# The first pair of heads: scores from raw float32 operands in place of rounded and split ones

## The chip, the cores and the metric

The kernel runs on one core of one Trainium2 chip. The metric is the device time of one execution in microseconds (us). The core has five engines that run their own instruction streams and meet only at semaphores: TensorE (PE in the profile; its weight loads are PEld), VectorE (DVE), ScalarE (ACT), GpSimd (POOL) and SyncE (SP), which here only issues DMA transfers. Each engine works strictly in the order of its own stream.

## What is computed

Windowed attention with a distance bias over 4 batches x 8 heads, sequence 576, head size 64, and then two feed-forward layers on the result.

```python
scores = scale * np.matmul(q, k.transpose(0, 1, 3, 2))
mask = (rel >= 0) & (rel < window)                      # window 128
scores = np.where(mask, scores + bias[None], -1000000000.0)
scores = scores - np.max(scores, axis=-1, keepdims=True)
attn = np.exp(scores)
attn = attn / (np.sum(attn, axis=-1, keepdims=True) + 1e-09)
x = np.matmul(attn, v)                                  # to (2304, 512)
h = x @ w_in;  g = h * (1.0 / (1.0 + np.exp(-1.702 * h)));  x = g @ w_out
h = x @ w_in2; g = where(h >= 1, h, where(h <= -1, 0, (h + 1) ** 2 / 4)); out = g @ w_out2
```

Inputs and output are float32, the weights 512 x 2048 and 2048 x 512 in each layer.

## The kernel before

**Stages.** Attention runs first, to about 146 us of the span; the two layers, built of three-term products of rounded and remainder parts, fill the rest. The change touches only the first pair of heads in attention.

**Attention.** The 32 heads are taken in 16 pairs. A pair has five steps (`ITEMS`): four of them hold two score blocks of 128 queries x 256 keys, the fifth (`d == 0`) both heads' tails of 64 queries. The order of the steps is `FIRST_ORDER = (2, 4, 3, 0, 1)` in the first pair and `STEP_ORDER = (2, 3, 0, 1, 4)` afterwards, so there are 80 steps, counted by `m`; steps 0 to 4 are the first pair's. For step m, TensorE makes the scores (line 994), VectorE adds the bias and finds the maximum (lines 1597, 1603), ScalarE takes exponentials (1225, 1230), TensorE transposes them two steps later (1007), ScalarE copies the result out of PSUM (1265), and TensorE multiplies with the values four or five steps after m (1022, 1028). Each engine's stream is written as a loop over m, and this loop is the order: what is placed at step m is queued behind everything of the steps before. Scores go round a ring of three PSUM banks.

**Operands.** A score product is made of rounded operands (fp32r). `qk_raw` holds four slots (`SPLIT_RING`) of raw queries and keys, head h in slot h % 4. In a slot, the upper 64 partitions hold both, the lower 64 the keys again, with zeros where the queries stand. VectorE rounds all of it into `qk_hi` (1579). The remainder of the keys goes to `k_lo`, by GpSimd (886), that of the queries to the lower half of `qk_hi`, by GpSimd too (890), for heads 2 and 3 by VectorE (1582). Two products, with `qk_hi` and with `k_lo`, then give a score block over 128 rows.

**The first pair.** Heads 0 and 1 are loaded in pieces (`load_piece`, lines 574 and 575: the upper half, then the keys for the lower half). The first piece has 384 keys (`FIRST_COLS`) and is rounded and split on VectorE (1554, 1556, 1563), ScalarE (1249, 1254) and GpSimd (872, 878); the rest follows (1569, 1571). Meanwhile TensorE runs products on zeros, `warm_up`: `WARM_UP = 22` ahead of step 0's scores and `KEEP_WARM = 16` behind them (line 967).

**Loads.** SyncE issues the transfers in a fixed order: pieces of heads 0 and 1, then heads 2 to 7 (`load_operands`, lines 584 and 586), each followed by the values (591, 592) of the head two before. Head 4 reuses slot 0, head 5 slot 1, so `load_operands` waits for the splits of heads 0 and 1. The identity for transposes and the tail part of the distance table are issued by ScalarE (1216, 1217). ScalarE makes the bias tables of pair 1 behind the exponentials of step 3 (`make_bias`, lines 1236 and 1243).

Of the kernel before, what the change touches and what calls it, by code (L numbers as in the profile page):

```python
# [58 lines left out]
WARM_UP = 22  # L59
KEEP_WARM = 16  # L60
# [26 lines left out]
CLEARED = 6  # L87
# [26 lines left out]
def build(nc, qkT, v_main, v_tail, w_pairs, bias_table, identity, out):  # L114
# [9 lines left out]
    def f32(ap):  # L124
        return ap.bitcast(F32)
# [50 lines left out]
    first_odd_rounded = sem("first_odd_rounded")  # L176
    first_rounded = sem("first_rounded")
    first_split = [sem(f"first_split{e}") for e in range(2)]
    first_keys_split = sem("first_keys_split")
    rest_rounded = sem("rest_rounded")  # L180
# [105 lines left out]
    def piece_keys(tile, e, first):  # L286
        if e == 0:
            return piece(tile, 0, first)[:, 0]
        keys_at = KEYS_AT[1] + FIRST_COLS
        return tile[:, 1, KEYS_AT[1]:keys_at] if first else tile[:, 1, keys_at:WIDTH]  # L290

    def piece_queries(tile, e, first, rows):
        return piece(tile, 0, first)[rows, 1] if e == 0 else all_queries(tile, 1, rows)

    def piece_lo(e, first):
        return k_lo[:, e, 0:FIRST_COLS] if first else k_lo[:, e, FIRST_COLS:SEQ]
# [267 lines left out]
    def _(sp):  # L564
        def load_piece(e, first):
# [5 lines left out]
            source_keys = qkT[e, :, SEQ * e:SEQ * (e + 1)]  # L571
            source_keys = source_keys[:, 0:FIRST_COLS] if first else source_keys[:, FIRST_COLS:SEQ]
# [173 lines left out]
        load_piece(1, True)  # L746
        load_piece(0, False)
# [121 lines left out]
    def _(pool):  # L869
        def split_first_keys():  # L870
            pool.wait_ge(first_odd_rounded, 1)
            nc.gpsimd.tensor_tensor(piece_lo(1, True), piece_keys(qk_raw, 1, True), f32(piece_keys(qk_hi, 1, True)),
                                    ALU.subtract).then_inc(first_keys_split, 1)
            pool.wait_ge(first_keys_split, 1)

        def split_rest_keys():
            pool.wait_ge(rest_rounded, 2)
            nc.gpsimd.tensor_tensor(piece_lo(1, False), piece_keys(qk_raw, 1, False), f32(piece_keys(qk_hi, 1, False)),
                                    ALU.subtract).then_inc(qk_split[1], 1)
            pool.wait_ge(qk_split[1], 1)  # L880

# [57 lines left out]
        split_first_keys()  # L939
        split_rest_keys()  # L940
# [22 lines left out]
    def _(pe):  # L963
# [5 lines left out]
        def scores(m):  # L969
            q, d = ORDER[m]  # L970
            if q == 0:
                if d == 2:
                    pe.wait_ge(first_split[0], 2)
                elif d == 4:
                    pe.wait_ge(first_split[1], 1)
                    pe.wait_ge(first_keys_split, 1)
                elif d == 3:
                    for head in (0, 1):
                        pe.wait_ge(qk_split[head], splits(head))
            elif d in (2, 3):  # L980
# [16 lines left out]

        def transpose_probs(m):
            q, d = ORDER[m]
            gi = group_of(m)  # L1000
# [210 lines left out]
    def _(act):  # L1211
# [21 lines left out]
        def make_bias(pair):  # L1233

            for h in (2 * pair, 2 * pair + 1):
                nc.scalar.activation(bias_sb[:, h], distance[:, 0:BAND], ACT.Copy, scale=SLOPES[h]).then_inc(bias_made, 1)
                if h == 0:
                    round_first(1)
                if pair == 0:
                    round_rest(h)  # L1240
            if pair == 0:
                act.wait_ge(tail_distance_in, 16)
# [3 lines left out]
        def round_first(e):  # L1246

            act.wait_ge(first_in[e], 32)
            nc.scalar.activation(piece(qk_hi, e, True), piece(qk_raw, e, True), ACT.Copy).then_inc(first_odd_rounded, 1)

        def round_rest(e):

            act.wait_ge(qk_in[e], 32)
            nc.scalar.activation(piece(qk_hi, e, False), piece(qk_raw, e, False), ACT.Copy).then_inc(rest_rounded, 1)
# [54 lines left out]
        for m in range(ALL_STEPS + TRANSPOSE_LAG):  # L1309
# [5 lines left out]
            if m in (3, 6, 11):  # L1315
                make_bias((3, 6, 11).index(m) + 1)
# [225 lines left out]
    def _(dve):  # L1542
# [4 lines left out]
        for e in range(2):  # L1547
# [465 lines left out]
```

## Time and profile before

| | |
|---|---|
| median of 3 runs | 856.34 us (856.2 to 856.57) |
| profiled execution | 856.35 us |
| its span, first to last instruction | 854.6 us |
| granted TensorE clock, mean | 1.000 |
| TensorE busy | 847.7 us, 99% |
| VectorE busy | 709.4 us, 83% |
| ScalarE busy | 537.0 us, 63% |
| GpSimd busy | 120.9 us, 14% |

The profile names an engine, the line of the kernel, the operation, and the tile written and read. Times of the trace count from the start of the span. A matmul's duration in it is the way of a product through the array, so that products that follow each other overlap: the distance from one start to the next is what a product costs. "Idle before" is the time in which the engine had nothing to run ahead of a row, and what ended it. TensorE is busy nearly all of the span, and the places at which it is not lie in the first 20 us.

### The profile page before, as it was taken

The page shows a single profiled execution, that of the slowest core. Times are in us where ns is not written, and L with a number is a line of the kernel's source. Part 1 is how long each engine was busy: PE and PEld are TensorE (multiplying, and loading weights), DVE is VectorE, ACT ScalarE, POOL GpSimd, SP SyncE. Part 2 cuts the span into 40 slices and gives each one's busy share as a digit, 9 for nine tenths or more (in the row PEclk, how much of TensorE's full clock was granted, in tenths as well). Part 3 has the DMA queues.
Part 4 walks back from the last instruction along what each step waited for, and adds up shares of the span by engine and source line. Part 5 has one row for each costly group of instructions (what it writes and reads, how often), then busy time and mean ns, then how long its engine had stood idle before and what let it go on. Part 6 is the DMA issues. An engine that isn't in the chain of part 4 may idle for free.

```text
span 854.6 us, 15515 instructions
## 1 busy us (share of the span) xinstructions
PE 847.7 (99%) x5746; PEld 844.2 (99%) x5746; DVE 709.4 (83%) x981; ACT 537.0 (63%) x789; POOL 120.9 (14%) x84
## 2 busy tenths in 40 slices
PE   8999999999999999999999999999999999999998
PEld 8999999999999999999999999999999999999998
DVE  7888988786988966778998887989989788889784
ACT  6778777767775546768644456767465567665441
POOL 5788898000000000000000000000000000000000
PEclk9999999999999999999999999999999999999999
DMA  8888761667776337686764772687647643788822
GB/s 204 220 211 219 199 170 67 267 256 270 258 246 232 129 144 271 253 306 244 259 243 177 279 242 104 219 284 259 230 143 278 226 156 122 287 302 299 302 74 75
DMA packets 63257, 186.45 MB, mean 218 GB/s; under 512 B 7504, under 2 KB 14352, under 8 KB 59344
## 3 DMA queue, kind: packets, MB, share of 16 engines
q1 hardware_dynamic: 62896, 185.30, 63.5%
q8 instruction: 47, 0.77, 0.4%
q14 instruction: 26, 0.21, 0.1%
q10 hardware_dynamic: 288, 0.16, 0.1%
HBM read 113.09 MB, written 72.35 MB: 217 GB/s over the span
## 4 chain that ended last, share of the span: by engine, by line
PE 95%; DVE 1%; SPq 1%; POOL 1%; issue 1%; DMA 0%; ACT 0%; DVEq 0%; POOLq 0%
PE ps L1060 83%; PE ps L1028 5%; PE ps L994 3%; PE ps L1007 3%; PE ps L1022 1%; PE ps L1037 1%; DVE qk_hi L1579 0%; DMA qk_raw<-qkT 0%; DVE probs L1603 0%; POOL qk_hi L890 0%; POOL k_lo L886 0%; SPq L575 0%; SPq L574 0%; DVE heads_out L1616 0%; PE ps L1042 0%
## 5 line engine op out<-in xcount | busy, mean ns | idle before, releaser
L1060 PE MATMUL ps<-arena,w_first 128*128 128x384 f32 x1764 | 331.3, 336 | 0.0
L1060 PEld LDWEIGHTS ps<-arena,w_first 128*128 128x128 f32 x1764 | 310.8, 188 | 0.9 <-DVE arena L1711 0.5
L1060 PE MATMUL ps<-arena,w_rest 128*128 128x384 f32 x1260 | 240.3, 336 | 0.0
L1060 PEld LDWEIGHTS ps<-arena,w_rest 128*128 128x128 f32 x1260 | 220.2, 188 | 0.5 <-issue 0.2
L1711 DVE TENSOR_TENSOR arena<-raw_first,arena 128x768 fp32r<-128x768 f32 (+1 forms) x114 | 148.8, 1318 | 77.2 <-ACT arena L1303 77.2
L1303 ACT ACTIVATE arena<-raw_first 128x768 fp32r<-128x768 f32 (+1 forms) x120 | 131.9, 1117 | 45.7 <-DVE raw_first L1672 39.7
L1060 PE MATMUL ps<-w_rest,arena 128*128 128x256 f32 x945 | 132.4, 281 | 0.0
L1060 PEld LDWEIGHTS ps<-w_rest,arena 128*128 128x128 f32 x945 | 121.1, 189 | 0.1
L1060 PE MATMUL ps<-w_first,arena 128*128 128x256 f32 x567 | 88.0, 282 | 0.0
L1711 DVE TENSOR_TENSOR arena<-raw_rest,arena 128x1536 fp32r<-128x1536 f32 (+1 forms) x48 | 71.3, 1486 | 8.6 <-ACT arena L1303 8.4
L1060 PEld LDWEIGHTS ps<-w_first,arena 128*128 128x128 f32 x567 | 76.0, 189 | 0.0
L1303 ACT ACTIVATE arena<-raw_rest 128x1536 fp32r<-128x1536 f32 (+1 forms) x48 | 60.9, 1268 | 23.0 <-PE ps L1060 21.0
L1345 ACT ACTIVATE d1s<-ps 128x384 f32<-128x384 f32 (+2 forms) x72 | 35.3, 490 | 40.9 <-PE ps L1060 40.8
L1230 ACT ACTIVATE probs<-probs,neg_max 128x256 f32<-128x256 f32 (+1 forms) x128 | 54.0, 472 | 7.4 <-DVE neg_max L1603 7.4
L1603 DVE CUSTOM_DVE_ANT_0 probs<-ps,bias_sb 128x256 f32<-128x256 f32 (+1 forms) x128 | 44.7, 387 | 16.0 <-PE ps L994 11.3
L1028 PE MATMUL ps<-v_sb,probs_t 128*128 128x65 f32 x448 | 57.0, 268 | 0.5 <-DVE heads_out L1616 0.5
L1028 PEld LDWEIGHTS ps<-v_sb,probs_t 128*128 128x128 f32 x448 | 55.3, 191 | 0.9 <-issue 0.9
L1336 ACT ACTIVATE ps<-ps 128x384 f32<-128x384 f32 (+2 forms) x72 | 34.2, 477 | 30.1 <-PE ps L1060 28.9
L1635 DVE TENSOR_TENSOR wst<-wst 128x256 f32<-128x256 f32 (+1 forms) x90 | 48.5, 538 | 2.8
L1265 ACT ACTIVATE probs_t<-ps 128x512 f32<-128x512 f32 x64 | 37.8, 590 | 18.8 <-PE ps L1007 18.8
L994 PE MATMUL ps<-qk_hi 128*128 128x256 f32 x160 | 48.6, 325 | 0.5 <-DVE qk_hi L1571 0.3
L886 POOL TENSOR_TENSOR k_lo<-qk_raw,qk_hi 128x576 fp32r<-128x576 f32 x30 | 44.7, 1490 | 16.9 <-DVE qk_hi L1579 15.6
(118 smaller groups left out, 973.1 us busy)
## 6 DMA issues: line engine op xcount, KB each, us to landing
gd<-g SPq DMA_DIRECT2D x24, 1536.0 KB, 6.1
raw_rest<-gd SPq DMA_DIRECT2D x32, 768.0 KB, 5.3
wst<-w_pairs SPq DMA_DIRECT2D x32, 512.0 KB, 5.8
raw_first<-gd SPq DMA_DIRECT2D x16, 768.0 KB, 5.9
yd<-ust SPq DMA_DIRECT2D x6, 1536.0 KB, 6.3
qk_raw<-qkT SPq DMA_DIRECT2D x30, 288.0 KB, 4.0
wd<-ust SPq DMA_DIRECT2D x4, 1536.0 KB, 9.4
raw_first<-yd SPq DMA_DIRECT2D x4, 1536.0 KB, 6.5
```

What stands on the lines that cost most here:

```text
L886: nc.gpsimd.tensor_tensor(k_lo[:, slot], keys(qk_raw, head), f32(keys(qk_hi, head)), ALU.subtract).then_inc(qk_split[slot], 1)
L994: last = nc.tensor.matmul(place, queries, k[:, key0:key0 + BAND], start=n_pass == 0 and (d > 0 or i == 0), stop=n_pass == 1 and (d > 0 or ...
L1028: last = nc.tensor.matmul(o_slot(2 * blk + e), probs_t[:, gi % 2, col:col + P], v_sb[:, h + e, max(blk - 1, 0) + piece], start=piece == 0, ...
L1060: last = nc.tensor.matmul(to, stationary, moving, start=start and n == 0, stop=n == len(steps) - 1, skip_group_check=True)
L1230: last = nc.scalar.activation(at, at, ACT.Exp, bias=neg_max[:, col:col + 1], scale=-1.0)
L1265: nc.scalar.activation(probs_t[:, gi % 2], pt_bank[gi % 2], ACT.Copy).then_inc(pt_copied[gi % 2], 1)
L1303: nc.scalar.activation(operand(k, i)[:, 0], source(k, i), ACT.Copy).then_inc(hi_made, 1)
L1336: nc.scalar.activation(b_bank(D, pos), a_bank(D, pos), ACT.Copy).then_inc(seeded_b, 1)
L1345: nc.scalar.activation(d1(D, pos), d_bank(D, pos), ACT.Copy).then_inc(d_copied, 1)
L1603: last = nc.vector.tensor_tensor_reduce(out=to[:, 0:width], in0=bank[:, i * BAND:i * BAND + width], in1=bias_sb[:, h + e, BAND - width:BAN ...
L1635: nc.vector.tensor_tensor(to, a, b, ALU.subtract).then_inc(w_added, 1)
L1711: nc.vector.tensor_tensor(at[:, 1], source(k, i), f32(at[:, 0]), ALU.subtract).then_inc(lo_made, 1)
```

## The change

The scores of the first pair's five steps are made straight from `qk_raw`, in float32, from the 64 upper partitions: one product a block instead of two. All rounding and splitting of heads 0 and 1 goes (on VectorE, ScalarE and GpSimd), and with it the four transfers of their lower halves. Products on zeros stand in front (14 instead of 22) and behind each of the five steps (3, 3, 4, 3, 3, instead of 16 behind step 0). SyncE issues the identity. Head 4's and head 5's loads now wait for the scores of the last step that reads heads 0 and 1. The order of some steps changes: the bias tables of pair 1 are made at step 2 instead of 3, the tail bias of pair 0 at step 1, and VectorE casts heads 2 and 3 at steps 2 and 3, with the query split of head 3 one step behind its cast.

```diff
-WARM_UP = 22
-KEEP_WARM = 16
+WARM_UP = 14
+KEEP_WARM = (3, 3, 4, 3, 3)
...
-CLEARED = 6
+CLEARED = 8
...
     def piece(tile, e, first):
-        ap = tile[:, e]
+        ap = tile[UPPER, e]
...
     def splits(head):
         use = head // SPLIT_RING
-        return 2 * use + 2 - (1 if head % SPLIT_RING == 1 else 0) if head >= 0 else 0
+        return 2 * use + 2 - (2 if head % SPLIT_RING < 2 else 0) if head >= 0 else 0
+
+    def landings(head):
+        return 32 * (head // SPLIT_RING + 1) - (16 if head % SPLIT_RING < 2 else 0)
...
-            sp.dma_start(piece(qk_raw, e, first)[UPPER], source_piece).then_inc(landed, 16)
-            sp.dma_start(piece_keys(qk_raw, e, first)[LOWER], source_keys).then_inc(landed, 16)
+            sp.dma_start(piece(qk_raw, e, first), source_piece).then_inc(landed, 16)
 
         def load_operands(head):
             slot = head % SPLIT_RING
             if head - SPLIT_RING in (0, 1):
-                sp.wait_ge(first_split[slot], 2 - slot)
-            if head - SPLIT_RING == 1:
-                sp.wait_ge(first_keys_split, 1)
+                sp.wait_ge(scores_ready, last_use(head - SPLIT_RING) + 1)
...
         load_piece(1, True)
+        sp.dma_start(ident[:], identity).then_inc(ident_in, 16)
         load_piece(0, False)
...
-        split_first_keys()
-        split_rest_keys()
         for head in range(2, 2 * PAIR_COUNT):
             split_head(head)
...
+        def first_scores(m):
+            d = ORDER[m][1]
+            if d == 2:
+                pe.wait_ge(cleared, CLEARED)
+                pe.wait_ge(first_in[0], 16)
+            elif d == 4:
+                pe.wait_ge(first_in[1], 16)
+            elif d == 3:
+                for head in (0, 1):
+                    pe.wait_ge(qk_in[head], landings(head))
+            wait_past(pe, scores_biased, m + 1 - SCORE_RING)
+            bank = score_bank[m % SCORE_RING]
+            for i, (e, blk) in enumerate(ITEMS[d] or ((0, 4), (1, 4))):
+                key0 = KEYS_AT[e] + (max(blk - 1, 0) * P if blk < 4 else SEQ - BAND)
+                query0 = QUERIES_AT[e] + blk * P if blk < 4 else TAIL_AT[e]
+                place = bank[:, i * BAND:(i + 1) * BAND] if d else bank[:, 0:BAND]
+                last = nc.tensor.matmul(place, qk_raw[UPPER, e, query0:query0 + P], qk_raw[UPPER, e, key0:key0 + BAND],
+                                        start=d > 0 or i == 0, stop=d > 0 or i == 1)
+            last.then_inc(scores_ready, 1)
...
         for m in range(ALL_STEPS + DRAIN):
-            if m < ALL_STEPS:
+            if m < STEPS:
+                first_scores(m)
+                warm_up(KEEP_WARM[m])
+            elif m < ALL_STEPS:
                 scores(m)
-            if m == 0:
-                warm_up(KEEP_WARM)
-                pe.wait_ge(ident_in, 16)
...
-        act.wait_ge(first_in[0], 32)
+        act.wait_ge(first_in[0], 16)
         act.dma_start(distance[:, BAND:], bias_table[:, BAND:]).then_inc(tail_distance_in, 16)
-        act.dma_start(ident[:], identity).then_inc(ident_in, 16)
...
-            if m in (3, 6, 11):
-                make_bias((3, 6, 11).index(m) + 1)
+            if m == 1:
+                act.wait_ge(tail_distance_in, 16)
+                make_tail_bias(0)
+            if m in (2, 6, 11):
+                make_bias((2, 6, 11).index(m) + 1)
+                make_tail_bias((2, 6, 11).index(m) + 1)
...
         for e in range(2):
+            nc.vector.memset(qk_raw[UPPER, e, ZEROS_AT[e]:ZEROS_AT[e] + TAIL], 0.0).then_inc(cleared, 1)
...
-        round_first()
         for m in range(ALL_STEPS + COPY_TAIL_LAG - 1):
...
-            if m == 0:
-                split_first_queries(1)
-                split_rest()
-            if m in (1, 2):
-                round_head(m + 1)
+            if m in (2, 3):
+                round_head(m)
+            if m in (2, 4):
+                split_queries(m // 2 + 1)
```

The order of TensorE's stream at its start, before the change. `arena` is the tile of zeros, `ps` is PSUM.

```order
L967 MATMUL ps<-arena 128x256 x21
L994 MATMUL ps<-qk_hi 128x256 [waits first_split0]
L994 MATMUL ps<-k_lo,qk_hi 128x256
L994 MATMUL ps<-qk_hi 128x256
L994 MATMUL ps<-k_lo,qk_hi 128x256
L967 MATMUL ps<-arena 128x256 x16
L994 MATMUL ps<-qk_hi 128x256 [waits first_keys_split,first_split1,ident_in]
```

And after the change, from the same place on to the first transposes.

```order
L938 MATMUL ps<-arena 128x256 x13
L977 MATMUL ps<-qk_raw 128x256 [waits first_in0,cleared]
L977 MATMUL ps<-qk_raw 128x256
L938 MATMUL ps<-arena 128x256 x3
L977 MATMUL ps<-qk_raw 128x256 [waits first_in1]
L977 MATMUL ps<-qk_raw 128x256
L938 MATMUL ps<-arena 128x256 x3
L977 MATMUL ps<-qk_raw 128x256 [waits qk_in1,qk_in0]
L977 MATMUL ps<-qk_raw 128x256
L938 MATMUL ps<-arena 128x256 x4
L992 MATMUL ps<-ident,probs 128x128 [waits probs_ready,ident_in]
```

A step has two products instead of four, they wait for transfers instead of splits, and the products on zeros stand behind every step.

The order of SyncE's stream from head 3's load (slot 3) to head 5's (slot 1), before the change.

```order
L584 DMA qk_raw<-qkT 64x1152
L586 DMA qk_raw<-qkT 64x576
L591 DMA v_sb<-v_main 128x260
L592 DMA v_sb<-v_tail 64x65
L584 DMA qk_raw<-qkT 64x1152 [waits qk_split0,first_split0]
L586 DMA qk_raw<-qkT 64x576
L591 DMA v_sb<-v_main 128x260
L592 DMA v_sb<-v_tail 64x65
L584 DMA qk_raw<-qkT 64x1152 [waits qk_split1,first_keys_split,first_split1]
```

And the same places after the change.

```order
L568 DMA qk_raw<-qkT 64x1152
L570 DMA qk_raw<-qkT 64x576
L575 DMA v_sb<-v_main 128x260
L576 DMA v_sb<-v_tail 64x65
L568 DMA qk_raw<-qkT 64x1152 [waits scores_ready]
L570 DMA qk_raw<-qkT 64x576
L575 DMA v_sb<-v_main 128x260
L576 DMA v_sb<-v_tail 64x65
L568 DMA qk_raw<-qkT 64x1152 [waits scores_ready]
```

The order stays, but heads 4 and 5 now wait for the fifth count of `scores_ready`, the scores of step 4; ahead of this piece stand 10 transfers instead of 13.

## Rows read from the trace of the kernel before

**Rows 1.** The page's busy times: us, share of the span, instructions.
```profile
PE 847.7 (99%) x5746; PEld 844.2 (99%) x5746; DVE 709.4 (83%) x981; ACT 537.0 (63%) x789; POOL 120.9 (14%) x84
```

**Rows 2.** TensorE's waits, whole run: line, releaser, us in total, times, longest.
```profile
PE ps L967 <- DVE arena L1544: 1.4, 1, 1.4
PE ps L1007 <- ACT probs L1230: 1.4, 2, 1.2
```

**Rows 3.** TensorE by time: start us, us, engine, line, operation, tiles, idle before.
```profile
1.36 5.06 PE L967 MATMUL ps<-arena 128*128 128x256 f32 x22 [1.36 <-DVE arena L1544]
6.22 0.47 PE L994 MATMUL ps<-qk_hi 128*128 128x256 f32 x1
...
7.13 2.18 PE L967 MATMUL ps<-arena 128*128 128x256 f32 x16
...
14.45 0.66 PE L1007 MATMUL ps<-ident,probs 128*128 128x128 f32 x4 [1.17 <-ACT probs L1230]
14.87 0.36 PE L994 MATMUL ps<-qk_hi 128*128 128x256 f32 x1
...
24.69 0.38 PE L994 MATMUL ps<-qk_hi 128*128 128x256 f32 x1
...
32.76 0.36 PE L994 MATMUL ps<-qk_hi 128*128 128x256 f32 x1
```

**Rows 4.** The chain that ended last, by time: start us, us, what.
```profile
9.49 4.01 DMA qk_raw<-qkT
13.52 1.03 DVE qk_hi L1579
```

**Rows 5.** VectorE by time, the casts of heads 4 and 5.
```profile
17.43 0.76 DVE L1579 CAST qk_hi<-qk_raw 128x1152 fp32r<-128x1152 f32 x1
...
18.95 1.43 DVE L1579 CAST qk_hi<-qk_raw 128x1152 fp32r<-128x1152 f32 x1
```

**Rows 6.** GpSimd by time, the splits of heads 4, 5 and 7.
```profile
18.33 1.43 POOL L886 TENSOR_TENSOR k_lo<-qk_raw,qk_hi 128x576 fp32r<-128x576 f32 x1 [1.73 <-DVE qk_hi L1579]
19.84 1.81 POOL L890 TENSOR_TENSOR qk_hi<-qk_raw,qk_hi 64x576 fp32r<-64x576 f32 x1
21.73 1.42 POOL L886 TENSOR_TENSOR k_lo<-qk_raw,qk_hi 128x576 fp32r<-128x576 f32 x1
23.23 1.41 POOL L890 TENSOR_TENSOR qk_hi<-qk_raw,qk_hi 64x576 fp32r<-64x576 f32 x1
...
30.27 1.42 POOL L890 TENSOR_TENSOR qk_hi<-qk_raw,qk_hi 64x576 fp32r<-64x576 f32 x1
```

**Rows 7.** Products with values, by line: ns min/median/max, first and last start, forms.
```profile
L1028 PE MATMUL ps<-v_sb,probs_t x448: 218/275/295, 15.4 to 144.2; 128*128 128x65 f32 x150
L1022 PE MATMUL ps<-v_sb,probs_t x64: 272/273/278, 20.7 to 142.7; 128*128 128x130 f32 x64
```

**Rows 8.** ScalarE by time, the first bias and the roundings of raw pieces.
```profile
5.56 0.42 ACT L1236 ACTIVATE bias_sb<-distance 128x256 f32<-128x256 f32 x1 [3.32 <-DMA distance<-bias_table]
6.57 1.01 ACT L1249 ACTIVATE qk_hi<-qk_raw 128x960 fp32r<-128x960 f32 x1 [0.60 <-DMA qk_raw<-qkT]
...
8.54 0.36 ACT L1254 ACTIVATE qk_hi<-qk_raw 128x192 fp32r<-128x192 f32 x1
```

**Rows 9.** Transfers: all to 40 us; SyncE by time; landing, lines 574, 575; lower halves.
```profile
DMA packets 5908, 8.67 MB, mean 217 GB/s; under 512 B 1699, under 2 KB 4195, under 8 KB 5904
...
0.75 0.67 SPq L574 DMA_DIRECT2D qk_raw<-qkT  x1
...
11.34 0.52 SPq L584 DMA_DIRECT2D qk_raw<-qkT  x1
...
DMA to landing us min/median/max: 2.7/3.2/3.2
...
DMA to landing us min/median/max: 2.7/3.0/3.3
...
qk_raw<-qkT SPq DMA_DIRECT2D x11, 144.0 KB, 4.6
```

More of the change, by code:

```diff
@@ L175, in build @@
     first_in = [sem(f"first_in{e}") for e in range(2)]
[L176 to L180, printed above, removed]
     v_in = [sem(f"v_in{i}") for i in range(HEADS)]
@@ L284, in piece @@
         return ap[:, TAIL:keys_at] if first else ap[:, keys_at:WIDTH]
[L286 to L296, printed above, removed]
     def splits(head):
         use = head // SPLIT_RING
-        return 2 * use + 2 - (1 if head % SPLIT_RING == 1 else 0) if head >= 0 else 0
+        return 2 * use + 2 - (2 if head % SPLIT_RING < 2 else 0) if head >= 0 else 0
+    def landings(head):
+        return 32 * (head // SPLIT_RING + 1) - (16 if head % SPLIT_RING < 2 else 0)
     def last_use(head):
@@ L970, in scores @@
             q, d = ORDER[m]
[L971 to L980, printed above, removed]
+            if d in (2, 3):
                 head = 2 * q if d == 2 else 2 * q + 1
@@ L996, in scores @@
             last.then_inc(scores_ready, 1)
+        def first_scores(m):
[17 more added lines that the diff above has]
+            last.then_inc(scores_ready, 1)
         def transpose_probs(m):
             q, d = ORDER[m]
+            if m == 0:
+                pe.wait_ge(ident_in, 16)
             gi = group_of(m)
@@ L1236, in make_bias, with make_tail_bias @@
                 nc.scalar.activation(bias_sb[:, h], distance[:, 0:BAND], ACT.Copy, scale=SLOPES[h]).then_inc(bias_made, 1)
[L1237 to L1242, printed above, removed]
+        def make_tail_bias(pair):
             nc.scalar.activation(bias_tail[:, pair], distance[:, BAND:BAND + TAIL_KEYS], ACT.Copy,
                                  scale=SLOPES[2 * pair]).then_inc(bias_made, 1)
[L1246 to L1254, printed above, removed]
         def copy_pair(q):
@@ L1547, in _ @@
         for e in range(2):
+            nc.vector.memset(qk_raw[UPPER, e, ZEROS_AT[e]:ZEROS_AT[e] + TAIL], 0.0).then_inc(cleared, 1)
             nc.vector.memset(f32(qk_hi[:, e::2, ZEROS_AT[e]:ZEROS_AT[e] + TAIL]), 0.0).then_inc(cleared, 1)
         nc.vector.memset(half[:], 0.5).then_inc(cleared, 1)
-        def round_first():
-            dve.wait_ge(first_in[0], 32)
-            nc.vector.tensor_copy(piece(qk_hi, 0, True), piece(qk_raw, 0, True)).then_inc(first_rounded, 1)
-            dve.wait_ge(first_rounded, 1)
-            nc.vector.tensor_tensor(piece_lo(0, True), piece_keys(qk_raw, 0, True), f32(piece_keys(qk_hi, 0, True)),
-                                    ALU.subtract).then_inc(first_split[0], 1)
-            split_first_queries(0)
-        def split_first_queries(e):
-            if e:
-                dve.wait_ge(first_odd_rounded, 1)
-            nc.vector.tensor_tensor(piece_queries(qk_hi, e, True, LOWER), piece_queries(qk_raw, e, True, UPPER),
-                                    f32(piece_queries(qk_hi, e, True, UPPER)), ALU.subtract).then_inc(first_split[e], 1)
-        def split_rest():
-            dve.wait_ge(rest_rounded, 1)
-            nc.vector.tensor_tensor(piece_lo(0, False), piece_keys(qk_raw, 0, False), f32(piece_keys(qk_hi, 0, False)),
-                                    ALU.subtract).then_inc(qk_split[0], 1)
-            nc.vector.tensor_tensor(piece_queries(qk_hi, 0, False, LOWER), piece_queries(qk_raw, 0, False, UPPER),
-                                    f32(piece_queries(qk_hi, 0, False, UPPER)), ALU.subtract).then_inc(qk_split[0], 1)
         def round_head(head):
             slot, use = head % SPLIT_RING, head // SPLIT_RING
-            dve.wait_ge(qk_in[slot], 32 * (use + 1))
+            dve.wait_ge(qk_in[slot], landings(head))
             if use:
@@ L1579, in round_head, with split_queries @@
             nc.vector.tensor_copy(loaded(qk_hi, head), loaded(qk_raw, head)).then_inc(qk_rounded, 1)
-            if head in DVE_QUERIES:
-                dve.wait_ge(qk_rounded, head - 1)
-                nc.vector.tensor_tensor(all_queries(qk_hi, head, LOWER), all_queries(qk_raw, head, UPPER),
-                                        f32(all_queries(qk_hi, head, UPPER)), ALU.subtract).then_inc(qk_split[slot], 1)
+        def split_queries(head):
+            dve.wait_ge(qk_rounded, head - 1)
+            nc.vector.tensor_tensor(all_queries(qk_hi, head, LOWER), all_queries(qk_raw, head, UPPER),
+                                    f32(all_queries(qk_hi, head, UPPER)), ALU.subtract).then_inc(qk_split[head % SPLIT_RING], 1)
         def bias_scores(m):
```

12 lines of the change are left out of this document (removed).

## The prediction

> **What bounds the kernel now.** I read the page's busy shares first: TensorE is busy 847.7 of 854.6 us [rows 1]. Then its waits over the whole run: of four entries the two longest are 1.4 us in front of the first product on zeros and 1.4 us in front of transposes that want probabilities [rows 2], both before 19 us; the other two hold 0.8 us together. So a change at the start is worth what it brings forward the point from which TensorE never waits again, and no more. The list by time shows that point [rows 3]. 22 products on zeros run from 1.36 us, the first scores start at 6.22, 16 more products on zeros fill 7.13 to 9.31, and the last long wait (1.17 us, for the exponentials of step 2) ends at 14.45. Step 5's scores, the first of pair 1, start at 14.87, those of step 11 at 24.69. Neither kind of filler is work; it covers loads, casts and splits.
>
> What ends that start late? Head 3's second transfer, issued at 9.49 as the fifteenth of SyncE's queue, takes 4.01 us and releases the cast at 13.52 [rows 4, 5]. Behind it stand head 4 and 5's casts (17.43, 18.95) and GpSimd's splits: head 4's k_lo at 18.33, its queries at 19.84, head 5's at 21.73 and 23.23, ending 24.64 [rows 5, 6]. Step 11's scores, which need head 5, start 0.05 us later. So there are two chains with next to no slack at 24.69: TensorE's own work, and GpSimd's. The second is simple arithmetic: from the end of head 4's cast (17.43 + 0.76 = 18.19) to the end of head 5's splits (24.64) are 6.45 us.
>
> **Price of a raw product.** There is no such product of 256 columns in the trace. Its kin are the products of probabilities with values, which are float32 too: 448 records for the 224 products of the code (14 per pair, 16 pairs), so two records a product. With 65 columns the shortest record is 218 ns, with 130 columns the median is 273 [rows 7]: 55 ns for 65 columns, 0.85 ns a column, two columns' time at the higher level of 2.4 GHz. At 256 columns a record then holds the array for 256 x 0.85 = 0.22 us and a step of two products, four records, for 0.88 us, against 4 x 0.118 = 0.47 us for the rounded pair it replaces (its records start 0.12 us apart once fast). Bounds: 0.47 us (columns cost nothing more) and 1.75 us (twice the records). I take 0.88; both kinds of evidence point at it. Five steps: 5 x 0.41 = 2.1 us more TensorE work. At the lower level, 1.2 GHz, where a product on zeros takes 4.86/22 = 0.221 us, it is 0.43 us a record.
>
> **The clock.** The granted clock of the rows reads 1.00 throughout, but pace tells which level holds: 0.221 us a product until about 7.1, then some 0.12 [rows 3]. TensorE had by then been busy without a gap since 1.36. I keep 7.3 us as the change, since the new kernel is as gapless.
>
> **TensorE's own chain after.** Removed are 8 of 22 products on zeros, and the wait for cast and two subtractions; 14 x 0.221 from 1.36 ends at 4.45. The first transfer of head 0 alone is needed: issued at 0.75, at most 3.2 us to land, 3.95, so it is there. Scores 0: 4 x 0.43, to 6.17. Three on zeros: 6.83. Scores 1 (second piece, issued near 2.1, landed by 5.3): one slow record, three fast, 7.92. Zeros 8.27, scores 2 9.15 (pieces issued by 3.9, landed by 7.1), four on zeros 9.62, transposes 10.02 (step 0's probabilities: VectorE from 6.5 to 7.3, ScalarE to 8.1; the identity, issued near 2.6, has landed). Scores 3 10.90, zeros 11.25, transposes 11.65, scores 4 12.53 with its result at 12.7; zeros and transposes to 13.3. Step 5's scores thus start at 13.3 instead of 14.87: 1.57 us won. For this the exponentials of steps 1 and 2 must be done by 11.25 and 12.9; they end near 9.8 and 11.6, behind VectorE's 0.7 us and ScalarE's 0.9 us a step. ScalarE also loses its three roundings of raw pieces (1.01 us the longest, 0.36 the shortest, 1.9 together [rows 8]); pair 1's biases move from behind step 3's exponentials to behind step 2's, about 1 us of work where it now has room. The distance table, issued 0.63 us earlier, lets the first bias start near 4.9 instead of 5.56 [rows 8].
>
> Heads 2 and 3: SyncE issues four lower-half transfers fewer and one (identity) more, three issues of about 0.63 us, 1.9 us earlier at head 3. It is also bytes: the transfers up to head 3 hold about 2.1 MB before and 0.29 MB less after, and the queue moves about 0.22 MB per us [rows 9], so head 3 lands near 11.7 to 12.1, is cast by 12.8 and its k_lo ready at 14.8; step 6's scores come at 15.7. That covers it; if it fails, each us is lost there.
>
> **The new wait.** SyncE now holds head 4's load for the scores of step 4, the last readers of the raw slots 0 and 1. Queued behind it are head 4's second half, head 2's values, head 5 and everything up to head 7. Before, head 4 was issued at 11.34 [rows 9]. After: 12.75, second half 13.4. Bounds of the landing: at the start, with an empty queue, second halves took 2.7 to 3.3 us; over the first 40 us, with a full queue, 4.6 at the median [rows 9]. Nothing was issued for 3.3 us before it, so I take the former, plus 0.2 for 144 instead of 96 KB: landed at 16.6 (bounds 16.1 and 18.0). Cast 0.76: done at 17.35, against 18.19, that is 0.84 us earlier (bounds 1.3 earlier, 0.6 later). Plus 6.45 gives 23.8 for step 11, where TensorE alone would come at 24.69 - 1.57 = 23.1. GpSimd decides: TensorE waits about 0.7 us and has won 24.69 - 23.8 = 0.9 us. The values and heads queued behind come 1.4 us later, but their need is far off (head 6 issued at about 17.5 for a cast near 24).
>
> What of head 5? Issued at 15.15 and 15.8, it lands at 18.9 (800 KB to 1 MB behind one another at 0.22 MB per us) or up to 20.4. The cast of head 5 took 1.43 us beside GpSimd's split instead of 0.76 [rows 5], and head 4's queries beside it 1.81 instead of 1.41 [rows 6]. If it lands inside head 4's query split, the two together end some 0.3 us later: 24.1. I take 0.1 of that: a gain of 0.8 us, on the profile's own 856.35 us (span 854.6 and 1.75 around it), equal to the median of 856.34. **Forecast 855.5 us.** After step 11 all is TensorE again: head 7's splits end at 30.27 + 1.42 = 31.69 and step 16's scores, which need them, start at 32.76 [rows 3, 6], 1 us of slack that the 0.8 us doesn't use up, so the gain goes through to the end unchanged.
>
> The Trainium skill ("SBUF — State Buffer", section "SBUF: two separate sides") says that VectorE and GpSimd share a port pair under an exclusive lock, so that whichever starts second waits for the whole of the other. The trace agrees with a cast that lasts until the split beside it has ended. By that rule head 5's cast would wait from 18.9 to the end of head 4's queries at 20.4.
>
> **Rivals.**
> (a) *Full lock on head 5's cast.* It waits until 20.4, ends at 21.2, and GpSimd's two further operations end at 24.1: gain 0.6, less 0.1 for step 7's bias that stands behind it: 855.8. For: the 1.43 us row [rows 5]; the rule of "SBUF — State Buffer" in the Trainium skill, told above, would make it so. Against: before, the cast came first and the split gave way.
> (b) *Earlier clock.* If the level rises at 4.8, 2.5 us of slow pace become 1.25, step 4 ends at 11.4, and head 4 follows: gain 0.8 + 1.25, 854.3. The same comes out if raw products cost less. For: nothing fixes the moment to 7.3. Against: one profile and three times within 0.4 us.
> (c) *Head 4's load takes the 4.6 us of the full queue.* Landed 18.0, cast 18.76, 0.57 us later than before: 856.9. For: most rows. Against: the queue is empty then.
> (d) *Slower: the clock stays at the lower level.* Raw products use 64 of 128 rows, and now stand among few products on zeros. If the pace of 0.221 lasts beyond 7.3, every us costs 0.5; gone at 9.0 is the whole gain, and with step 4 all slow, 5.4 us are added at 12.7, less 0.8: 860.9. For: 20 records of a kind the trace has not. Against: no gap opens for it.
> (e) *Raw products need more records than two*, or fewer, against what the 448 records say: a step of 1.75 us would add 5 x 0.87 = 4.4 us before the end of step 4 and lead to about 860, one of 0.47 us lead to (b)'s time.
>
> **Chances.** Forecast 0.35 (own range 855.0 to 855.8), (a) 0.15, (b) 0.20, (c) 0.16, (d) 0.09, (e) 0.05. A measurement of this kernel can tell about 0.2%, 1.7 us. Faster than 854.6: most of (b) and half of (e), 0.19. Slower than 858.1: (d), half of (e) less a little, 0.12. Within: 0.69. The range leaves out (d) and the ends of (b) and (c): 854.1 to 857.5.
>
> **What would show it.** Right: the first raw product at 4.4 to 4.5, records 0.43 us apart and after 7.3 us 0.22 apart; step 4's scores ending near 12.7, head 4's transfer issued at once, its cast ending near 17.4; a wait of about 0.7 us of TensorE on GpSimd's split before step 11, at 23.8. Wrong: that wait missing or longer; a cast of head 3 that comes after 12.8; SyncE not idle between 9.4 and 12.7; pace 0.22 for products on zeros after 8 us; or two records of a raw product not 0.22 us apart.

## The result, and the profile after

The changed kernel is slower: 858.9 us at the median of 10 runs, against 856.4 of the kernel before (ratio 1.0051, 95% interval 1.0035 to 1.0066). That is half a per cent, and clear of the noise. Its times are not one cluster. Over the 16 times measured of it in this study, 8 lie at 864.09 to 864.71, 6 at 858.55 to 859.01, and 2 at 857.1 and 857.7; the kernel before lies at 855.97 to 857.00. Three executions of this study (1004 and 1391 us of the kernel before, 2148 us of own128nf below) lie far outside and stand in no comparison. A median between such clusters says little, so two traces are shown: the profiled run, at 864.51 us (span 862.7), and one more of the same kernel, look2, at 858.82 (span 857.0).

First the waits of TensorE in the run at 864.51: line, releaser, us in total, times, longest.

```profile
PE ps L938 <- DVE arena L1518: 1.4, 1, 1.4
PE ps L1013 <- DVE heads_out L1570: 0.8, 3, 0.3
```

It waits less than before: the 1.17 us for probabilities [rows 2, 3] are gone, as forecast. The time went elsewhere. TensorE by time in the same run (start us, us, engine, line, operation, tiles, count):

```profile
1.36 3.36 PE L938 MATMUL ps<-arena 128*128 128x256 f32 x14 [1.36 <-DVE arena L1518]
4.65 2.07 PE L977 MATMUL ps<-qk_raw 64*128 64x256 f32 x4
6.65 1.01 PE L938 MATMUL ps<-arena 128*128 128x256 f32 x3
7.59 2.07 PE L977 MATMUL ps<-qk_raw 64*128 64x256 f32 x4
...
18.33 2.07 PE L977 MATMUL ps<-qk_raw 64*128 64x256 f32 x4
20.33 1.01 PE L938 MATMUL ps<-arena 128*128 128x256 f32 x3
21.14 1.05 PE L992 MATMUL ps<-ident,probs 128*128 128x128 f32 x4
21.84 0.56 PE L956 MATMUL ps<-qk_hi 128*128 128x256 f32 x1
...
25.23 0.36 PE L956 MATMUL ps<-qk_hi 128*128 128x256 f32 x1
...
32.88 0.36 PE L956 MATMUL ps<-qk_hi 128*128 128x256 f32 x1
```

The first raw product starts at 4.65, as it should. But every raw step costs 2.0 us, and the pace of the lower level (1.2 GHz) lasts until 23.9 us, though TensorE is never idle in that time. Before, it ended at 7.4: between the products on zeros that start at 7.34 and 7.48 the distance falls from 0.21 us to 0.14, and then to 0.12. The trace's own first record of the granted clock lies at the same places, 23.91 and 7.36 us. Step 5's scores come at 21.84 instead of 14.87, and step 11's at 32.88 instead of 24.69 [rows 3]: 8.19 us, against 8.16 us in the time. All of it was lost by step 11.

Now look2, 858.82 us, TensorE's waits and its list by time:

```profile
PE ps L992 <- ACT probs_tail L1209: 1.6, 1, 1.6
```

```profile
4.61 1.13 PE L977 MATMUL ps<-qk_raw 64*128 64x256 f32 x4
5.67 0.62 PE L938 MATMUL ps<-arena 128*128 128x256 f32 x3
6.21 1.13 PE L977 MATMUL ps<-qk_raw 64*128 64x256 f32 x4
...
13.90 0.37 PE L956 MATMUL ps<-qk_hi 128*128 128x256 f32 x1
...
22.91 0.44 PE L992 MATMUL ps<-ident,probs_tail 128*128 128x128 f32 x2 [1.61 <-ACT probs_tail L1209]
...
26.21 0.56 PE L956 MATMUL ps<-qk_hi 128*128 128x256 f32 x1
```

Here the clock is up before the first raw product, at 4.51 us, and step 5's scores come at 13.90, 1 us ahead of before. Then TensorE waits 1.61 us for the exponentials of step 7. Who is late? VectorE's casts of heads 4 and 5 in look2:

```profile
17.66 0.76 DVE L1531 CAST qk_hi<-qk_raw 128x1152 fp32r<-128x1152 f32 x1 [1.41 <-DMA qk_raw<-qkT]
...
20.85 1.24 DVE L1531 CAST qk_hi<-qk_raw 128x1152 fp32r<-128x1152 f32 x1 [1.75 <-DMA qk_raw<-qkT]
22.02 0.34 DVE L1551 CUSTOM_DVE_ANT_0 probs_tail<-ps,bias_tail 128x192 f32<-128x192 f32 x1
```

GpSimd's split beside the second cast:

```profile
20.06 1.42 POOL L863 TENSOR_TENSOR qk_hi<-qk_raw,qk_hi 64x576 fp32r<-64x576 f32 x1
```

and SyncE's issues of their transfers (upper half, then keys for the lower half):

```profile
13.19 0.47 SPq L568 DMA_DIRECT2D qk_raw<-qkT  x1
13.70 0.60 SPq L570 DMA_DIRECT2D qk_raw<-qkT  x1
...
15.48 0.59 SPq L568 DMA_DIRECT2D qk_raw<-qkT  x1
16.11 0.60 SPq L570 DMA_DIRECT2D qk_raw<-qkT  x1
```

Head 4 is issued at 13.19 instead of 11.34 [rows 9]. Head 5's second half, issued at 16.11, is awaited until 20.85, 4.7 us; step 7's bias stands behind its cast. Before, that cast ran at 18.95 without a wait [rows 5]. Half a microsecond of the delay is GpSimd's: the cast takes 0.76 us alone and 1.24 here, since it lasts until 0.6 us behind the split that was running when it began. And the wait has a second cost, in the granted clock (columns: stretch, its length, TensorE's busy time and instructions, granted clock, DMA share, GB/s):

```profile
24.00:25.00 1.00, 0.88 (x8) 1.00 0.98 205
25.00:26.00 1.00, 1.00 (x7) 0.50 1.05 252
26.00:27.00 1.00, 1.00 (x7) 0.50 0.68 169
27.00:28.00 1.00, 1.00 (x7) 0.50 0.73 114
28.00:29.00 1.00, 1.00 (x10) 0.80 0.93 288
```

The clock falls to the lower level from 25.0 to about 28.4, behind the wait: 3.4 us at half pace are 1.7 us lost. So there are two separate losses: a rise of the clock that is missed (the times at 864), and SyncE's wait with the fall behind it (those at 858.8).

### The profile page after: what moved, and what is told of

The parts are those of the page before. It is cut to its first block, busy times and chain, and to the rows that moved or that the text cites. A ratio compares the mean times of both kernels' runs of the same rounds, so it can differ in the third digit from the quotient of the medians.

```text
span 862.7 us, 15483 instructions
## 1 busy us (share of the span) xinstructions
PE 857.4 (99%) x5738; PEld 849.0 (98%) x5738; DVE 704.6 (82%) x977; ACT 535.4 (62%) x786; POOL 118.3 (14%) x82
## 4 chain that ended last, share of the span: by engine, by line
PE 96%; DVE 2%; POOL 1%; DMA 1%; issue 1%; SPq 0%; DVEq 0%; POOLq 0%
PE ps L1045 82%; PE ps L1013 4%; PE ps L956 3%; PE ps L992 3%; PE ps L977 1%; PE ps L938 1%; PE ps L1007 1%; PE ps L1022 1%; DMA qk_raw<-qkT 1%; DVE probs L1557 0%; POOL qk_hi L863 0%; DVE qk_hi L1531 0%; POOL k_lo L859 0%; DVE heads_out L1570 0%; PE ps L1027 0%
## 5 line engine op out<-in xcount | busy, mean ns | idle before, releaser
L1235 ACT ACTIVATE probs_t<-ps 128x512 f32<-128x512 f32 x64 | 37.8, 591 | 28.0 <-PE ps L992 22.8
L956 PE MATMUL ps<-qk_hi 128*128 128x256 f32 x150 | 45.7, 326 | 0.1
```

What stands on the lines that cost most here:

```text
L956: last = nc.tensor.matmul(place, queries, k[:, key0:key0 + BAND], start=n_pass == 0 and (d > 0 or i == 0), stop=n_pass == 1 and (d > 0 or ...
L1235: nc.scalar.activation(probs_t[:, gi % 2], pt_bank[gi % 2], ACT.Copy).then_inc(pt_copied[gi % 2], 1)
```

## The experiments

### What keeps the clock down: rows, kind, or number of products

**warm64.** The kernel before, its products on zeros over 64 partitions.

```diff
-                nc.tensor.matmul(ps[:, 5, 0:BAND], arena[:, 0:P], arena[:, P:P + BAND], start=True, stop=True)
+                nc.tensor.matmul(ps[:, 5, 0:BAND], arena[UPPER, 0:P], arena[UPPER, P:P + BAND], start=True, stop=True)
```

> The kernel before, with its 38 products on zeros made over the 64 upper partitions instead of 128 (still fp32r, 256 columns, 0.221 us each at the lower level). If products over 64 rows are what keeps the clock at the lower level, the pace stays near 0.22 us past 7.3 us, step 1's scores start some 1 to 1.5 us later than 9.39 and the time spreads or rises by 0.5 to 6 us over 856.4. If the float32 kind is the cause, or only the number of products ahead, nothing changes: pace 0.12 from 7.1 to 7.3 us, 856.4 within 0.3.

Measured: 858.64 us (858.60 to 858.81), ratio 1.0025 (1.0016 to 1.0035). TensorE by time:

```profile
7.52 3.78 PE L967 MATMUL ps<-arena 64*128 64x256 f32 x16
11.23 0.58 PE L994 MATMUL ps<-qk_hi 128*128 128x256 f32 x1
```

16 products take 3.78 us, all at the lower pace, where before they took 2.18 [rows 3]; the higher pace comes near 15.9 us. Nothing else was changed: half the rows alone put off the rise. It also lies far outside the moments at which the clock rose in any trace with full-height products in front (4.5 to 7.4 us, listed below).

**warmf32.** The kernel before, its products on zeros in float32 over all rows.

```diff
-WARM_UP = 22
-KEEP_WARM = 16
+WARM_UP = 6
+KEEP_WARM = 4
-                nc.tensor.matmul(ps[:, 5, 0:BAND], arena[:, 0:P], arena[:, P:P + BAND], start=True, stop=True)
+                nc.tensor.matmul(ps[:, 5, 0:BAND], f32(arena[:, 0:P]), f32(arena[:, P:P + BAND]), start=True, stop=True)
```

> The kernel before, with its products on zeros made in float32 over all 128 partitions, 6 and 4 of them (two records each, so about the same time at the lower level as 22 and 16). If the float32 kind keeps the clock down, the pace stays at the lower level past 7.3 us and the time rises by 0.5 to 6 us. If the 64 rows are the cause, nothing changes: the pace rises near 7.2 us, 856.4 within 0.5.

Measured: 856.42 us, ratio 1.0000 (0.999 to 1.0009). The float32 kind does not keep the clock down: in the trace it rises at 4.74 us, earlier than the 7.2 expected, and the time does not move, since waits for casts and probabilities take up what is won. The run also gives the price at full height: 8 records, of which the last starts 1.51 us after the first, 0.216 us each at the higher level, as the prediction read from [rows 7].

**raw128.** The changed kernel, raw products over all rows, the lower half cleared to zeros.

```diff
+                pe.wait_ge(raw_cleared, 2)
-                last = nc.tensor.matmul(place, qk_raw[UPPER, e, query0:query0 + P], qk_raw[UPPER, e, key0:key0 + BAND],
+                last = nc.tensor.matmul(place, qk_raw[:, e, query0:query0 + P], qk_raw[:, e, key0:key0 + BAND],
-            nc.gpsimd.memset(qk_raw[LOWER, e::2, (SEQ, TAIL)[e]:(SEQ, TAIL)[e] + SEQ], 0.0).then_inc(raw_cleared, 1)
+            nc.gpsimd.memset(qk_raw[LOWER, e], 0.0).then_inc(raw_cleared, 1)
+        for e in range(2):
+            nc.gpsimd.memset(qk_raw[LOWER, 2 + e, (SEQ, TAIL)[e]:(SEQ, TAIL)[e] + SEQ], 0.0).then_inc(raw_cleared, 1)
```

> The changed kernel, with its raw products over all 128 partitions, the lower 64 of them zeros (GpSimd clears two more stretches). If the 64 rows keep the clock down, it now rises between 5 and 9 us in every execution, records of raw products come 0.22 us apart, step 4's scores end near 12.7, and the time is 855.5 (854.1 to 857.5) without modes. If rows of zeros do not count, or the float32 kind is the cause, nothing changes: modes at 857 to 864.5, median near 859.

Measured: 858.59 us (856.13 to 860.89), ratio 1.0023 (1.0011 to 1.0035). Half right. The times at 864 are gone, and step 5's scores come at 12.67, earlier than the 13.3 forecast. But the time is not 855.5. TensorE's longest wait:

```profile
PE ps L995 <- ACT probs_tail L1212: 1.7, 1, 1.7
```

and the granted clock behind it:

```profile
20.00:23.00 3.00, 1.16 (x9) 1.00 0.87 213
23.00:24.00 1.00, 0.85 (x4) 0.52 0.96 230
24.00:30.00 6.00, 6.00 (x31) 0.51 0.87 211
30.00:36.00 6.00, 6.00 (x57) 1.00 1.05 249
```

It is some 7 us at half pace. The ten executions fall into three groups by their mean granted clock: 856.13 to 856.58 us at 1.000 (three), 858.48 to 858.59 at 0.998 (three), 859.59 to 860.89 at 0.996 (four). A mean of 0.998 is 3.4 us at half pace, one of 0.996 twice that. So the fall costs 2 to 4 us, and is not there in three of the ten. This is the run that showed the second cause.

**warm30.** The changed kernel with `WARM_UP = 30`.

> The changed kernel with 30 products on zeros ahead of step 0 instead of 14 (2.5 to 3.5 us more of filler). If only the rise was missed, the clock has risen by 7.2 us, before the first raw product, and stays up: step 4's scores end near 7.2 + 0.3 + 6.6 = 14, and the time is 856.5 to 857.5 in every execution. If the raw products themselves count for too little, the clock falls back among them and modes up to 862 or more remain.

Measured: 859.78 to 863.46 us in four runs, median 861.27, ratio 1.005 (1.0033 to 1.0067), not the 856.5 to 857.5 expected. The clock was up at the first raw step (7.39 us) and stayed up through all five, so that half of the expectation was right; but the 1.7 us wait before step 7's transposes is there, the granted clock's mean is 0.996 in two of the four, the traced one among them, and the 2.7 us of later start were not given back.

### What SyncE's wait costs

**own128, own64, own128nf.** The first pair gets a tile of its own (in `raw_first`, which is free at that time), so that heads 4 and 5 wait for nothing. own64 does this to the changed kernel, own128 to raw128, and own128nf is own128 with `KEEP_WARM = (0, 0, 0, 0, 0)`.

```diff
+    first_raw = raw_first[:].rearrange("p a b -> p (a b)")[:, 0:2 * WIDTH].rearrange("p (e w) -> p e w", e=2)
+    rest_in = [ctx.enter_context(nc.semaphore(f"rest_in{e}")) for e in range(2)]
...
-            landed = first_in[e] if first else qk_in[e]
-            sp.dma_start(piece(qk_raw, e, first), source_piece).then_inc(landed, 16)
+            landed = first_in[e] if first else rest_in[e]
+            sp.dma_start(piece(first_raw, e, first), source_piece).then_inc(landed, 16)
...
-            if head - SPLIT_RING in (0, 1):
-                sp.wait_ge(scores_ready, last_use(head - SPLIT_RING) + 1)
```

> The changed kernel with raw products over 128 partitions (the lower 64 zeros) and the first pair in a tile of its own, so that heads 4 and 5 no longer wait for the scores of step 4. If those two waits (the thin products and SyncE's) are the whole of the loss: head 4's transfer is issued at 9.3 to 9.4 instead of 12.16, head 5's at 11.8, the cast of head 5 does not wait, TensorE has no wait at step 7's transposes and the clock does not fall: 854.0 to 855.0 in every execution. If the clock's fall at 23 us had another cause, modes up to 861 remain.

> The changed kernel with only SyncE's two waits undone (a tile of its own for the first pair), raw products over 64 partitions as in the change. If the thin products keep the clock down by themselves, step 4's scores still end at 16 to 20 us, TensorE has no wait for step 7's probabilities, and the time is 857 to 862, in modes. If SyncE's wait was the main loss, the time is near 855.

> As own128, without the 16 products on zeros behind the first five steps. If the filler only fills, step 5's scores wait for head 2's split instead and the time is that of own128 or up to 1 us less (16 x 0.12 = 1.9 us of TensorE work go). If filler is needed to hold the clock up, gaps open among the first steps, the rise comes later than in own128 and the time goes up by 1 us or more, in modes.

Measured: own128 855.13 us (854.55 to 855.51), ratio 0.9985 (0.9976 to 0.9995). own64 855.08 to 855.72 in 8 runs, 864.06 and 864.09 in two, ratio 1.0008 (0.9979 to 1.0038). own128nf 854.86 us, ratio 0.9981 (0.997 to 0.9991). The median of own128 is 0.1 us above what was expected of it, and its wait before step 7's transposes and the fall are gone.

With both causes out, the rest of the change gains 1.2 us. In own128 what is left in front of step 11 is a wait for what the prediction named, GpSimd's split of head 5, 0.55 us:

```profile
23.41 0.39 PE L956 MATMUL ps<-qk_hi 128*128 128x256 f32 x1 [0.55 <-POOL qk_hi L862]
```

own64 separates the two: taking SyncE's wait away moves the cluster of times at 858.8 to a median of 855.25 (3.5 us), and leaves times at 864. The filler behind the steps is not needed at full height: without it the clock rises as well (6.45 us in the trace), and step 5's scores wait 0.58 us for head 2's split instead, as expected.

**swap128.** raw128, with head 5's load issued ahead of head 2's values.

```diff
-        for h in range(2, HEADS):
+        for h in range(2, 6):
             load_operands(h)
-            load_values(h - 2)
+            if h < 4:
+                load_values(h - 2)
+        load_values(2)
+        load_values(3)
+        for h in range(6, HEADS):
+            load_operands(h)
+            load_values(h - 2)
```

> The kernel raw128 with one change: SyncE issues head 5's load ahead of the values of head 2, right behind head 4's. If the cast of head 5, waiting for its transfer, is what stops TensorE at step 7's transposes (1.68 us), its two transfers come 1.2 us earlier, the wait falls to about 0.5 us, and the median falls from 858.6 to between 855.5 and 857. If the wait comes from elsewhere it stays at 1.7 and so do the modes.

Measured: 855.69 us (855.40 to 856.37), ratio 0.9992 (0.9983 to 1.0002); the wait is 0.51 us instead of 1.68, and the mean granted clock 1.000 instead of 0.996. Issuing head 5's two transfers 1.1 us sooner behind head 4's gives back 2.9: most of the wait, and the clock's fall. So it is head 5's transfer that TensorE waits for in the end.

**waitonly.** The kernel before, with SyncE's wait added.

```diff
                 sp.wait_ge(first_split[slot], 2 - slot)
+                sp.wait_ge(scores_ready, last_use(head - SPLIT_RING) + 1)
```

> The kernel before with one thing of the change: head 4's and head 5's loads wait for the scores of step 4 as well. Those end near 13.1, so head 4 is issued at 13.2 instead of 11.34. If this wait is a loss of its own: head 5's transfer, issued near 16.1 and landing some 5 us behind, holds VectorE's cast until 21 to 21.5 instead of 18.95, step 7's probabilities come late, TensorE waits 0.5 to 1 us there, the clock falls in some executions, and the time is 857.5 to 860. By my step in the prediction (3.2 us to land, GpSimd's split decides) it would be 856.4 to 857.2.

Measured: 857.43 us (856.64 to 858.16), ratio 1.0011 (1.0002 to 1.0021), between the two ranges named, and just short of the one for a loss (857.5 to 860). Head 4 was issued at 13.59 and cast at 18.01; head 5's cast began at 20.96 instead of 18.95 [rows 5] and TensorE waited 0.44 us before step 7's transposes. In the profiled run the clock does not fall behind so short a wait. SyncE's wait costs 1 us in the kernel before, where TensorE comes to step 7's transposes at 22.8, and 3.5 in the changed one, where it comes at 21.3.

### When the raw products begin

**own64w22, warm22.** 22 products on zeros ahead of step 0 instead of 14, in own64 and in the changed kernel.

> The kernel own64 with 22 products on zeros ahead of step 0 instead of 14. If the slow mode (864.1) comes from raw products over 64 rows that begin before the clock has risen, the mode is gone or rarer, and the rest is 855.5 to 856.5 (8 x 0.22 = 1.8 us more filler, part of it beside loads). If it has nothing to do with when they begin, 2 in 10 stay at 864.

> The changed kernel with 22 products on zeros ahead of step 0 instead of 14, SyncE's wait kept. The clock should have risen before the raw products in every execution, as in own64w22, so that what is left over own64w22 (856.86) is SyncE's wait alone: TensorE waits 1.5 to 1.8 us in front of step 7's transposes, the pace behind it falls to the lower level for some us in some or all executions, and the times are 858.5 to 861.5. Without the wait being a cause they would be those of own64w22.

Measured: own64w22 856.86 us (855.95 to 857.41), ratio 1.0003 (0.9994 to 1.0013), no time at 864 in 10. warm22 860.09 us (859.92 to 861.31, four runs), ratio 1.0047 (1.003 to 1.0063), none either, 1.57 us of wait before step 7's transposes in its trace and a mean granted clock of 0.996 to 0.998 in all four. The difference of the two, 3.2 us, is SyncE's wait once more.

The rise is missed with 14 products ahead in 10 of 26 times (changed kernel and own64 together), with 22 or 30 ahead in none of 18. The traces point at what sets the two apart. All of them begin at 1.36 us with gapless products on zeros over all rows, warm64 aside, and yet the clock rises at a different moment in each. Where the rise was not missed it lies at 4.51 us (look2), 4.74 (warmf32), 4.78 (own64), 5.14 (warm22), 5.78 (waitonly), 5.96 (raw128), 6.25 (best), 6.41 (own128), 6.45 (own128nf), 6.49 (warm30), 6.57 (swap128), 6.66 (own64w22) and 7.36 (before). The products over 64 rows begin at 4.6 in the changed kernel. In the two traces that escaped, the rise came by then (4.51, and 4.78 against a first raw product at 4.65); in the three others (after, again, look3) it had not, and came at 23.9 to 24.3. In own64w22 it still came 0.3 us behind the first product over 64 rows, so a few of those do not prevent it; what becomes of a rise as late as 7.36 us with 22 products ahead, no trace shows.

**again, look2, look3.** The changed kernel as it is.

> The changed kernel once more, for a trace of its commoner mode and for the shares of the modes. If the two causes are as found, times lie at 864.4 (clock at the lower level until some 22 us) and at 857 to 859; a trace of the latter has raw steps 1.6 us apart, a wait of about 1.7 us in front of step 7's transposes, and the lower pace behind it for some us. If the lower mode had another cause, its trace shows no such wait.

> The changed kernel, one more trace. If it falls into the commoner mode (857 to 859), it shows a gap of 1.5 to 1.8 us in front of step 7's transposes and the lower pace behind it; if into 864.4, the raw products and all until some 22 us at the lower pace, and no gap.

> The changed kernel, one more trace, with the same expectation as look2: by the shares so far about half of the executions are of the commoner mode.

Measured: again 864.50, 858.75, 864.09, 864.62 us, with a trace of a time at 864; look2 858.82, the trace shown above, as expected; look3 864.71.

### A version that beats both

**best.** own128nf, with head 4's query split on VectorE.

```diff
-DVE_QUERIES = (2, 3)
+DVE_QUERIES = (2, 3, 4)
...
                     round_head(head)
+                    if head == 4:
+                        split_queries(4)
```

> The kernel own128nf, with head 4's query split on VectorE behind its cast, so that GpSimd comes to head 5 1.4 to 1.9 us earlier. If GpSimd's chain to head 5 is what TensorE waits for at step 11 (0.54 us), that wait goes and the time is 854.2 to 854.6; if VectorE's 0.75 us more delays step 6's bias instead, 854.9 or a little more.

Measured: 854.80 us (854.60 to 855.71), ratio 0.9983 (0.9974 to 0.9992), the same as own128nf. TensorE's wait for GpSimd at step 11 is gone, and a new one of 0.56 us, for step 7's exponentials, has taken its place: VectorE's 0.75 us stand in front of step 6's and 7's biases. own128nf, 854.86 us, is the simplest version that beats the kernel before, by 1.5 us.

## Why the prediction was wrong

**Direction and range.** It said 855.5 us (854.1 to 857.5), a gain of 0.8 us. The median is 858.9. The missed rise was named as rival (d), with a chance of 0.09 and a loss of 4.6 us; it took half of the executions and cost 8. A late load was rival (c), with 0.16 and 856.9, but for head 4, where the one that TensorE waited for was head 5's. That the clock could fall again behind a wait stood in no rival.

**Step "the clock": failed.** "I keep 7.3 us as the change, since the new kernel is as gapless." Gapless it is. But that was not enough: warm64 shows that products over half the rows put the rise off from 7.4 to 15.9 us, and in the times at 864 it came at 23.9 to 24.3. Rival (d) said just this and was set at 0.09 because "no gap opens for it". Where a kind of work had no row in the trace, the point at which the whole price hung deserved more than that. Nor is 7.3 us a fixed moment. One profile gave it, and in the 12 other traces without a missed rise it came 0.7 to 2.9 us earlier. In look2 the condition of rival (b), a rise at 4.8 us, was met, and SyncE's wait took all it gave.

**Term "raw product": 0.88 us a step, mis-sized for this height.** At full height the record is 0.22 us, as read from two lines' durations. Over 64 rows the records in the middle of a step are no dearer, but the changes of height are. A step and its three fillers take 6.30 to 7.91, 1.61 us, in own64, where own128 needs 6.71 to 7.92, 1.21:

```profile
6.30 1.13 PE L976 MATMUL ps<-raw_first 64*128 64x256 f32 x4
7.36 0.62 PE L937 MATMUL ps<-arena 128*128 128x256 f32 x3
7.91 1.13 PE L976 MATMUL ps<-raw_first 64*128 64x256 f32 x4
```

```profile
6.71 1.03 PE L978 MATMUL ps<-raw_first 128*128 128x256 f32 x4
7.38 0.71 PE L938 MATMUL ps<-arena 128*128 128x256 f32 x3
7.92 1.03 PE L978 MATMUL ps<-raw_first 128*128 128x256 f32 x4
```

The weight loads of own64 between 3 and 14 us sit idle at these places (line, releaser, us, times, longest), and those of own128 do not:

```profile
PEld ps L937 <- issue: 1.7, 5, 0.3
PEld ps L976 <- issue: 0.4, 2, 0.2
```

This fits a weight load that is not made ahead of its product where the height changes; no run shows that reason by itself. Five steps of 0.4 us are 2 us that the sum did not hold. At the lower level a raw step took 2.0 us instead of 1.72.

**Step "the new wait": the place was wrong.** For head 4, 3.2 us from issue to landing were assumed, with an empty queue; look2 shows 13.70 to 17.66, 4.0 us. For head 5, 18.9 to 20.4 was the forecast, with step 4 ending at 12.7; it was 20.85 with step 4 ending at 13.2, so that this size was right near its late end. The failure is in what stands behind: "GpSimd decides", the prediction said. Step 7's bias, which stands behind head 5's cast, had no term in its sum, and 0.1 us in rival (a). In truth VectorE does not reach that bias until the cast is through, and TensorE reaches step 7's transposes at 21.3, ahead of step 11, and waits there for 1.61 us. The rows of VectorE were read for the cast, not for the next instruction behind it.

**Rival (a), the lock, is in the traces.** The exclusive lock that the Trainium skill tells of ("SBUF — State Buffer", "SBUF: two separate sides") was its rule. The traces agree. Wherever head 5's cast begins beside a split that GpSimd had begun before it, the cast ends 0.61 to 0.62 us behind that split, whenever it began: it took 1.43 us before, 1.24 in look2, 1.59 in own128, 1.07 in swap128, 0.83 in raw128. The prediction held against this rival that the cast had come first before; GpSimd's first split, at 18.33 [rows 6], had begun before the cast at 18.95 [rows 5], and only the second gave way. In look2 the lock's 0.5 us lie on the way to TensorE's wait, where rival (a) looked for it at step 11.

**What held, and what was luck.** The 1.17 us wait went. TensorE's own chain was priced rightly at full height: own128 comes to step 5's scores at 12.94, and the forecast of 13.3, less the half of the 0.9 us by which its clock rose earlier, is 12.85. The 13.90 of look2 is near 13.3 only because two errors offset each other: 2.0 us for the changes of height, and 1.4 us won by a clock that rose at 4.5 instead of 7.3. GpSimd's 6.45 us from the end of head 4's cast to the end of head 5's splits is 6.46 in own128 (16.90 to 23.36). But that own128 lies 0.4 us from the forecast does not bear out the new wait: that kernel has none, and head 4's cast there waits for no transfer.

**Left open.** The two times of 857.1 and 857.7 have no trace; their mean granted clock is 1.000, where those at 858.55 to 859.01 have 0.998, so they are probably executions in which the clock did not fall behind the wait, as raw128 has three. Why the clock rises anywhere from 4.5 to 7.4 us behind the same products isn't shown by any run, nor why it falls behind a wait in some executions only.

## What to carry to other kernels

Ask of every product at the start of a kernel how many rows it uses, not only whether it leaves gaps: keep it full height, with zeros in the unused rows, or begin it only when the clock is up. Do not build on the moment at which one profile shows the clock rising. When a load is made to wait, follow the queue to the last load behind it, and on the engine that consumes it to the next instruction behind the consumer; that is the one that comes late. A kernel whose times fall into modes needs a trace of each before it is explained.

## What was new about the hardware

- Products over 64 of 128 rows put off the rise of TensorE's clock, on zeros in fp32r (warm64: 15.9 instead of 7.4 us) as on data in float32 with full-height ones between them (after, again, look3: 23.9 to 24.3 us); float32 over all rows does not (warmf32: 4.74 us). Rows that hold zeros count (raw128 and the others at full height: no time at 864 in 50).
- With gapless full-height products on zeros from 1.36 us on, the clock rose at moments from 4.51 us (look2) to 7.36 us (before).
- The granted clock of the rows reads 1.00 at the start of a run even where the pace is that of the lower level, since the trace's first record of the clock is the rise itself; warm64's trace has no record at all. At the start, only the distance between products tells, or that first record.
- A wait of 1.6 to 1.7 us and one of 0.3 us behind it were followed by a fall of the clock in each of the four traces that had them (raw128, warm30, warm22, look2), for 3.4 or 6.8 us at half pace. Waits of 0.4 to 0.6 us were not (waitonly, own128, swap128, best). The mean granted clock says that some executions of raw128 (three of ten) and of warm30 (two of four) had no fall; they have no trace.
- A step over 64 rows with three full-height products behind it took 1.61 us, one over 128 rows 1.21 (own64, own128).
- A cast on VectorE beside a split that GpSimd had begun before it ended 0.61 to 0.62 us behind that split, in before, look2, own128, swap128, raw128 and waitonly; alone it takes 0.76 us.
